# Attention and two gated layers on one core: staged queries, values by three steps, and other orders in the second groups

## What is computed

```python
scores = where(mask, scale * q @ k.T + bias, -1e9)      # 128 keys back from each query
x = softmax(scores) @ v                                 # to 2304 x 512
x = (sigmoid(x @ w_gate) * (x @ w_val)) @ w_out
out = ((x @ w1) * (x @ w2)) @ w3 @ moe2_w_out
```

## Time and profile before

| | |
|---|---|
| median of 3 runs | 878.67 us |
| the profiled execution | 878.12 us |
| its span on the core | 876.3 us |
| mean granted clock of TensorE | 0.998 |
| busy: PE, POOL, DVE, ACT | 98%, 68%, 59%, 54% |
| DMA | 78.79 MB, mean 90 GB/s |

### The profile page before, as it was taken

The page is one execution under the profiler, slowest core; times in us unless marked ns, Lnnn a source line. Parts: engine busy times, 40 slices in busy tenths (PEclk is TensorE's granted clock), DMA queues, the critical chain, the costliest instruction groups (busy, mean ns, idle before and its releaser), DMA issues.

```text
span 876.3 us, 15447 instructions
## 1 busy us (share of the span) xinstructions
PE 860.5 (98%) x5272; PEld 824.8 (94%) x5272; DVE 514.7 (59%) x1209; ACT 473.3 (54%) x1043; POOL 593.9 (68%) x502
## 2 busy tenths in 40 slices
PE   5999999999999999999999999999999999999998
PEld 4887999999999999999999999999999999999998
DVE  5563665655467646666456656555776555576554
ACT  6566675666656644668555565733544444345330
POOL 3449588666655986759866663896859867648930
PEclk9999999999999999999999999999999999999999
DMA  8465323304222033341332122222231222212202
GB/s 245 132 196 162 109 94 104 100 13 122 83 80 92 25 105 99 101 141 39 98 113 87 50 80 80 73 73 73 82 110 33 90 73 73 73 49 73 73 25 73
DMA packets 59453, 78.79 MB, mean 90 GB/s; under 512 B 23152, under 2 KB 40688, under 8 KB 59376
## 3 DMA queue, kind: packets, MB, share of 16 engines
q1 hardware_dynamic: 58432, 77.52, 28.0%
q10 hardware_dynamic: 944, 0.30, 0.1%
HBM read 70.98 MB, written 6.82 MB: 89 GB/s over the span
## 4 chain that ended last, share of the span: by engine, by line
PE 89%; POOL 4%; ACT 2%; DVE 2%; issue 2%; SPq 1%; DMA 1%; ACTq 0%; DVEq 0%; POOLq 0%
PE quad_ps L610 15%; PE quad_ps L612 15%; PE quad_ps L611 15%; PE o_ps L610 11%; PE o_ps L612 11%; PE o_ps L611 11%; PE attn_ps L668 4%; PE attn_ps L633 3%; PE attn_ps L648 2%; PE quad_ps L633 1%; POOL wq_lo L1297 1%; PE quad_ps L648 1%; POOL wq_lo L1290 1%; DMA w_raw<-w3t 1%; POOL w_lo L1314 1%
## 5 line engine op out<-in xcount | busy, mean ns | idle before, releaser
L610 PE MATMUL quad_ps<-xs_hi,wq_hi 128*128 128x384 f32 x840 | 291.4, 347 | 1.1 <-DVE quad_ps L1057 0.5
L612 PE MATMUL quad_ps<-xs_hi,wq_lo 128*128 128x384 f32 x840 | 281.4, 335 | 0.0
L611 PE MATMUL quad_ps<-xs_lo,wq_hi 128*128 128x384 f32 x840 | 281.1, 335 | 0.0
L610 PE MATMUL o_ps<-h_hi,wo_hi 128*128 128x384 f32 x480 | 166.2, 346 | 0.6 <-DVE xf L1096 0.3
L610 PEld LDWEIGHTS quad_ps<-xs_hi,wq_hi 128*128 128x128 f32 x840 | 157.8, 188 | 6.8 <-issue 2.6
L612 PE MATMUL o_ps<-h_hi,wo_lo 128*128 128x384 f32 x480 | 161.2, 336 | 0.0
L611 PE MATMUL o_ps<-h_lo,wo_hi 128*128 128x384 f32 x480 | 161.0, 335 | 0.0
L611 PEld LDWEIGHTS quad_ps<-xs_lo,wq_hi 128*128 128x128 f32 x840 | 158.0, 188 | 0.0
L612 PEld LDWEIGHTS quad_ps<-xs_hi,wq_lo 128*128 128x128 f32 x840 | 157.7, 188 | 0.0
L1253 POOL TENSOR_TENSOR soft<-soft,recip 128x384 f32<-128x384 f32 (+2 forms) x80 | 58.4, 730 | 146.3 <-DVE recip L999 146.2
L1297 POOL TENSOR_TENSOR wq_lo<-wsum,wq_hi 128x1024 fp32r<-128x1024 f32 x60 | 144.4, 2407 | 8.5
(11 more groups left out here) (68 smaller groups left out, 1361.2 us busy)
## 6 DMA issues: line engine op xcount, KB each, us to landing
raw_q<-w SPq DMA_DIRECT2D x24, 512.0 KB, 3.5
raw_q<-w_gate SPq DMA_DIRECT2D x18, 512.0 KB, 3.5
raw_q<-w_val SPq DMA_DIRECT2D x18, 512.0 KB, 4.7
wo_lo_raw<-w_out SPq DMA_DIRECT2D x18, 512.0 KB, 4.1
wo_lo_raw<-w_times_wout SPq DMA_DIRECT2D x12, 512.0 KB, 4.0
w_raw<-w3t SPq DMA_DIRECT2D x16, 256.0 KB, 3.2
outT<-xf SPq DMA_DIRECT2D x8, 384.0 KB, 3.5
q_sb<-qT SPq DMA_DIRECT2D x30, 96.0 KB, 3.4
```

The costliest lines, as they stand in the source:

```text
L610: pe.matmul(out, lh, rh, start=start, stop=False, skip_group_check=onto)
L611: pe.matmul(out, lh, rl, start=False, stop=False, skip_group_check=onto)
L612: return pe.matmul(out, ll, rh, start=False, stop=stop, skip_group_check=onto)
```

## The change

**Opening.** The queries of jobs 0 and 1 (a job is a batch's two heads over 2 or 3 steps) are loaded in one DMA each, as they lie, into two buffers not yet in use, and DVE copies them to their places (two copies each). On SP's queue the second half of w3 is issued ahead of the fifth block of the second factor and of the first values. GpSimd, not ACT, casts that half, in slot 2, before it scales a step. DVE splits the factor's blocks at the head of a slot and in other slots. A fold issues its two matmuls on the high part of w3 before it waits for the low part.

**Values.** `pv` runs for three steps at a time (`VALUES`), in the head in slots 6, 9, 12, ... and after it in each third section, with three `pt` buffers; the copies out take the steps of one job together. Loads of values follow the end of such a three.

**Second groups.** ACT casts the plain weights first, then keeps P1, then hidden C21; DVE takes the low part of C12 before hidden C21; GpSimd scales the step ahead of the weight sums in val.

```diff
-WO2_LO_SLOT = by_slot([1 + r // 2 if r else -1 for r in range(IB)])
+WO2_LO_SLOT = by_slot([-1, 1, 2, 2, 3, 4, 4, 5])
+VALUES = [list(range(a, min(a + 3, end))) for lo, end in ((0, HEAD), (HEAD, NSTEP)) for a in range(lo, end, 3)]
+VALUES_BY_JOB = [[[n for n in ns if STEP[n][0] == j] for j in sorted({STEP[n][0] for n in ns})] for ns in VALUES]
+VALUES_AT = {ns[-1]: i for i, ns in enumerate(VALUES)}
+        q_stage = xt[0:2]
-        pt = [sb(ctx, f"pt{b}", [P, 4 * P], F32) for b in range(2)]
+        pt = [sb(ctx, f"pt{b}", [P, 4 * P], F32) for b in range(3)]
@@ sync
-            load_q(1)
+            sp.dma_start(q_stage[1][:, 0:queries(1)], qT[...]).then_inc(stage_in[1], 16)
             load_wo2(2)
             load_wo2(3)
+            load_w3(1)
+            load_wo2(4)
             load_v(0)
-            load_wo2(4)
-            load_w3(1)
@@ tensor, scores
-                    pe.wait_ge(x_ready, n - 1 if n == HEAD else (n - 1) // 2 * 2)
+                    pe.wait_ge(x_ready, VALUES[VALUES_OF[n - 1]][0])
@@ tensor, pv
-                    wait(pe, x_ready, n - 1)
+                    wait(pe, x_ready, VALUES[VALUES_OF[n] - 1][0] if VALUES_OF[n] else 0)
@@ tensor, fold
+                if r % 4 == 0:
+                    w3_high_wait(pe, hf)
+                if m == 0:
+                    pe.wait_ge(wo2_hi_done, r + 1)
...
+                pe.matmul(bank, w3_hi[hf % 4][:, w], wo2_hi[:, cols], start=r == 0, stop=False)
+                if m == 0:
+                    pe.wait_ge(wo2_split, r + 1)
+                pe.matmul(bank, w3_hi[hf % 4][:, w], wo2_lo[:, cols], start=False, stop=False)
                 if r % 4 == 0:
                     pe.wait_ge(w3_split, hf + 1)
+                mm = pe.matmul(bank, w3_lo[hf % 4][:, w], wo2_hi[:, cols], start=False, stop=r == IB - 1)
@@ tensor, slots (and likewise in the sections)
-                if 0 <= s - LAG_PV < HEAD and s % 2:
-                    pv(s - LAG_PV - 1)
-                    pv(s - LAG_PV)
+                if s - LAG_PV in VALUES_AT:
+                    for n in VALUES[VALUES_AT[s - LAG_PV]]:
+                        pv(n)
@@ scalar
-                for n in (last - 1, last):
-                    nc.scalar.copy(out_cols(n), pv_cols(n)).then_inc(x_ready, 1)
+                for ns in VALUES_BY_JOB[VALUES_AT[last]]:
+                    nc.scalar.copy(out_cols(ns), pv_cols(ns)).then_inc(x_ready, len(ns))
@@ scalar, gate of a second group
                     if g and first_of(g - 1):
+                        plain_hi(g, 1)
+                    keep(2 * g)
+                    if g and first_of(g - 1):
                         hidden_hi(g - 1, C21)
-                    keep(2 * g)
...
-                    weights_hi(g, 1)
+                    sums_hi(g, 1)
@@ vector
+            def place_queries(j):
+                dve.wait_ge(stage_in[j], 16)
+                for h in range(2):
+                    src = q_stage[j][h * U:(h + 1) * U, 0:queries(j)].rearrange("p (u n) -> p u n", n=U)
+                    nc.vector.tensor_copy(q_units(j, h, h, queries(j) // U), src).then_inc(q_placed, 1)
...
+            place_queries(0)
             wo2_low(0)
...
+                if s == 0:
+                    place_queries(1)
...
                     if g and first_of(g - 1):
+                        hidden_lo(g - 1, C12)
                         hidden(g - 1, C21)
-                        hidden_lo(g - 1, C12)
@@ gpsimd
+                if s == 2:
+                    pool.wait_ge(w3_in[1], 16)
+                    nc.gpsimd.tensor_copy(w3_hi[1][:, :], w3_raw[1][:, :]).then_inc(w3_hi_1, 1)
...
                     out_lo(g)
+                    if n is not None and first_of(g - 1):
+                        normalise(n)
                     if more:
                         weight_sums(g + 1, 1)
-                    if n is not None:
+                    if n is not None and not first_of(g - 1):
                         normalise(n)
```

More of the change, by code:

```diff
@@ L201, in loads_to, with query_loads_to @@
     return sum(set_of(i) == set_of(j) for i in range(j + 1))
+def query_loads_to(j):
+    return sum(set_of(i) == set_of(j) for i in range(2, j + 1))
 def value_loads_to(j):
@@ L585, in _ @@
                         load_q(j)
-                    if end_of(before(j, v_set)) > HEAD and sec == end_of(before(j, v_set)) + 1 - HEAD:
+                    if end_of(before(j, v_set)) > HEAD and sec == values_end(before(j, v_set)) + 2 - HEAD:
                         load_v(j)
@@ L769, in _ @@
                             turn(m)
-                        if j == P7 and m is not None and m % 2:
-                            pv(m - 1)
-                            pv(m)
+                        if j == P7 and m in VALUES_AT:
+                            for n in VALUES[VALUES_AT[m]]:
+                                pv(n)
                 else:
@@ L785, in _ @@
                             turn(m)
-                        if i == 5 and m is not None and m % 2:
-                            pv(m - 1)
-                            pv(m)
+                        if i == 5 and m in VALUES_AT:
+                            for n in VALUES[VALUES_AT[m]]:
+                                pv(n)
         @block.scalar
@@ L815, in turned_copy @@
                 act.wait_ge(turned, n + 1)
-                wait(act, pv_done, n - 1)
-                nc.scalar.copy(cols(pt[n % 2]), cols(turn_bank(n))).then_inc(pt_done, 1)
+                wait(act, pv_done, n - 2)
+                nc.scalar.copy(cols(pt[n % 3]), cols(turn_bank(n))).then_inc(pt_done, 1)
             def x_hi(inst, j):
@@ L943, in _ @@
                     gate(g, C11)
-                    if m is not None and m % 2:
+                    if m in VALUES_AT:
                         out_copies(m)
@@ L1115, in _ @@
             for s in range(SLOTS + 1):
+                for r in WO2_LO_SLOT.get(s, ()):
+                    wo2_low(r)
                 if 0 <= s - LAG_TURN < HEAD:
```

71 lines of the change are left out of this document (41 added, 30 removed).

## The result

The changed kernel takes 867.41 us (median of 4, 867.13 to 867.92), the kernel before beside it 878.57 (876.58 to 879.76): a ratio of 0.9876, interval 0.9857 to 0.9895. It is 11.2 us faster; forecast were 9.15 us, 869.5, and the range of 866.0 to 873.5 holds the time.

A forecast was written before the change was run, and what follows sets the result against it. PE, busy 98% of the span, was taken as the bound. Gains of 1.5 + 3.2 + 0.8 + 0.2 + 0.45 + 3.0 = 9.15 us gave 869.5 us, range 866.0 to 873.5.

The forecast's parts named there:

- The opening: First 20 us: earlier scores and w3's second half bring the fold forward; 1.5 us gained, bounds 0.3 and 3.5.
- rival B: At 18 to 21 us the half-speed clock goes too: up to 1.5 us more, 868.0; chance 0.12.
- Rival A: Opening gives nothing: DVE's order and a lock against POOL's cast hold the folds; 871.0 us, chance 0.15.
- Values by three: Value products after the head: 8 fewer groups, each saving a 0.40 us change of kind; 3.2 us gained.
- rival C: Value products: the change of kind is paid by the step, so threes save nothing; 873.5 us, chance 0.06.
- 8 groups x 0.40 = 3.2: Main part's value products: 18 groups in place of 26, each change of kind costing 0.40 us whatever its steps.
- rival D: Main groups: next section's scores wait for copies after three steps; slower, 883.0 us at 0.75 each, chance 0.04.
- The head: Before the main part: 0.8 us from fewer value groups, 0.2 from a copy wait, 0.45 from the fold's wait.
- one gap of four: Head's value groups: 0.3 us taken off for the gap between 64 and 80 us, where POOL sets the time.
- Second groups: Waits in groups 21, 27 (1.7 us together), 17 (0.7) and 1 (0.6) go: 3.0 us, between 1.5 and 3.5.
- late in its place: Second groups: hidden C21's high part comes 1.3 us later, near 657.9, before P7 needs it at 658.5.
- Rival E: Second groups exchange one wait for another (P7 on hidden C21); 871.2 us, chance 0.11.

The follow-up runs named there:

- the fours: Changed kernel with value products for four steps at a time in the main part (13 groups) and a fourth `pt` buffer: 867.02 us.
- the threes in proj and in gate: Changed kernel, main part's threes begun after a first group of one step (most in proj, 869.04 us) or of two (most in gate, 871.28 us).
- the singles: Changed kernel with value products for one step at a time in the main part (52 groups in place of 18): 879.77 us.
- the pairs kernel: Changed kernel with value products for two steps at a time again (40 groups instead of 28): 870.74 us.
- ScalarE's run: Changed kernel with only ACT's old order in the second groups (hidden C21, keep, then plain and sum weights together): 873.33 us.
- the first four experiments: The first four follow-up kernels, with the kernel before beside them at 877.58 us.

## Why the prediction came out right

**The opening** (forecast 1.5, measured 1.8 at equal clock, 2.2 in the medians). The signs came: first scores near 5 us (4.7), the fold of 17.47 at about 16 (16.23), and step 1's exponentials earlier by 2.1 us where 1.3 was counted. But the fold's date agrees in part by luck. The forecast had it follow POOL's low part. That part was done 1.9 us earlier (15.51 for 17.41), and the fold was set by PE, which started at half rate and stayed there until 14.13 us. In the profiles of the fours and of the threes in proj and in gate, which have the same opening, the 512-column distances are down to 0.23 or 0.24 by 12.4 us; there this fold starts at 13.7 to 14.6, and its third matmul waits for the low part until 14.8 to 15.7. That PE begins at half rate was in none of the forecast's terms. The unknown durations were well bounded: a copy to place queries took 0.37 (0.4 taken), POOL's cast 1.07 (1.0 taken). What the sum left out was the low clock, which was rival B, forecast as 1.5 us for certain with a chance of 0.12. It was right that the low clock goes, and wrong on the certainty: 1.5 us in half of the executions, 0.7 us on average. That the idle time of PE is what brings the low clock isn't shown: the threes-only kernel's profile had PE idle for 1.10 us until 17.81 and kept its clock. The forecast and B were never alternatives; the clock term should have stood in the sum at its half.

Rival A fell. What it rested on was there, but small: at 11.03 two splits on DVE took 1.80 us beside POOL's cast, in place of 1.38, so the meeting cost 0.42, not the 1.0 of its bound. By the Trainium skill (SBUF — State Buffer, section on SBUF's two separate sides) the instruction that comes second waits for the whole of the other. The rows fit that nearly: DVE's second split ended 0.55 us after POOL's instruction (12.83 and 12.28 here, 17.96 and 17.41 in the earlier trace rows), where a free split takes 0.69. The loss is less than POOL's recorded length because that length seems to hold POOL's own wait for DVE's first split; no run shows the cast without DVE beside it.

**Values by three** (forecast 3.2 in the main part, measured 3.3). That it is paid by the group was right, and the singles end rival C. The price was read somewhat high: 0.40 a group from the earlier trace rows, 0.31 by the singles without their other waits, 0.23 to 0.32 in the table above. The Trainium skill (TensorEngine Tiling (Array Packing), section on key properties) says that a change of tiling mode drains TensorE; it gives no time, and the rows here put 0.25 ahead and 0.17 behind a group of 64-column tiles. But the step "8 groups x 0.40 = 3.2", taken as the whole of the effect, failed: fours, with five groups fewer still, gave nothing, and threes in other sections gave 1.0 or -0.5. Most of the changed kernel's threes (14 of 18) lie in val, where they cover DVE's work ahead of proj, and that is worth some 1.5 of the 3.3. The forecast looked at the copies (rival D) as what could be late, and not at what the products' own 1.5 us hide or uncover for DVE. That all this came to 3.3 is in good part luck: a price too high by about as much as the term that was left out.

**The head** (0.8 + 0.2 + 0.45): threes alone on the kernel before gave 1.3 there, where 1.0 was forecast with the copy wait; undone last, in the pairs kernel, they show nothing clear of the 1.2 us by which heads differ. The gaps are gone as counted, yet PE still waits 0.33 us in the fold for POOL's low part near 76.5 us (its weight load 0.76):

```profile
76.53 0.19 PEld L726 LDWEIGHTS o_ps<-wo_hi,w_lo 128*128 128x128 f32 x1 [0.76 <-POOL w_lo L1370]
```

POOL's date may take back what was won ahead of it, as the forecast allowed for one gap of four; for the rest that is argued from this row, not shown.

**Second groups** (forecast 3.0, measured 3.5 to 4.0). Groups 21 and 27: forecast 0.86 each, 0.93 between the two traces, 0.9 undone. Group 17's 0.7 came to 0.67 by the distance of its two matmuls between the two traces, but undoing the order costs only 0.4. What was mis-sized is groups 1 and 11. For group 1 the orders were counted at 0.2 (the rest of its 0.6 is the scores' wait, which the threes remove), for group 11 at nothing; undone they cost 0.7 each. With the old orders PE waits for a sigmoid there, 0.5 us more than in the changed kernel in group 1 and 0.3 more in group 11. The reasoning on DVE's place for C12 held alone (0.5 a group), but it was incomplete: it called hidden C21 "late in its place" and asked only whether P7 would wait. ScalarE's run shows that the late one is whatever ACT has behind C21. Rival E didn't come: P7 waits for hidden C21 in neither group.

**The sum.** Forecast 9.15. Against the medians of the kernel before on the chips used, the changed kernel's median is 10.2 to 11.2 us lower. The undone parts sum to 3.3 + 2.2 + 3.5 = 9.0; the 1.3 by which threes are worth more on the old kernel make 10.3, against 877.58 - 867.41 = 10.2 (the kernel before on the chip of the first four experiments). The 1.3, in the head, stay without a cause.

Rival D (slower) had nothing for it: scores no longer wait for copies anywhere.

## What to carry to other kernels

Group small matmuls of another shape to pay their change of kind less often, but choose the group's length and phase so that it falls ahead of the section that would otherwise wait for another engine; test the phase with the number held fixed. When two engines work through one list of steps, change their orders together: one order alone can cost more than neither. And where a profile shows a stretch at half clock, look at the clocks of all executions before pricing it, and check the distance of equal matmuls too: the clock column didn't show the half rate at the start.

## What the runs showed of the hardware that was not expected

The low stretch is decided anew in each execution: 15 of 32 executions of one unchanged program had a lower mean clock and were some 1.5 us longer. In the profile of before PE had idled 1.09 us until 17.47, in that of the old opening 1.47 until 15.68 and 1.09 until 17.43, and the clock fell with the work that came next. In the threes-only kernel's profile the queries landed as late (7.78 us, 7.84 before) and PE idled 1.10 until 17.81, yet its clock stayed at 1.00; it fell in two other executions of the five.

PE starts at half rate in every profile here, and when it rises varies between profiles of one opening: in the changed kernel's the 512-column distances fall from 0.42 to 0.23 us at 14.1 to 14.5 us, in that of the fours they are at 0.23 at 11.5. PE had begun at 4.7 to 4.8 in both, and the column of the granted clock says 1.00 throughout.

One DMA of whole rows against two of 64-number runs: queue 10 moved the same 0.30 MB in 288 packets in place of 944, and the first queries landed 4 us earlier in the profile (3.85 for 7.84). The scores began 3.2 us earlier, 2.9 were forecast. Over all profiles the old loads landed at 6.6 to 7.8 us, the new one at 3.9 to 4.1.
